# An attention order with early loads, an eviction and a maximum exchanged, and three splits of x moved one tile earlier

## What is computed

```python
scores = scale * np.matmul(q, k.transpose(0, 1, 3, 2))
scores = np.where(causal, -1000000000.0, scores)
scores = scores - scores.max(-1, keepdims=True)
a = np.exp(scores)
a /= a.sum(-1, keepdims=True) + 1e-09
local = np.matmul(a, v)
...
mem_ret = np.einsum('bhsd,bhde->bhse', q_p, M_prev)
mem_norm = np.einsum('bhsd,bhd->bhs', q_p, z_prev)[..., None] + 1e-06
mem_out = mem_ret / mem_norm
g = 1.0 / (1.0 + np.exp(-beta))[None, :, None, None]
return (g * mem_out + (1 - g) * local).astype(np.float32)
...
h = x @ w_in
g = np.where(pos, h, np.where(neg, 0.0, (h + beta) ** 2 / (4.0 * beta)))
return (g @ w_out).astype(np.float32)
...
h = x @ w_in
g = h * (1.0 / (1.0 + np.exp(-h)))
return (g @ w_out).astype(np.float32)
```

## Time and profile before

| what | value |
|---|---|
| median of the runs | 1012.22 us |
| lowest and highest | 1009.32 and 1012.91 us |
| the profiled execution | 1008.85 us |
| its span | 1006.8 us |
| granted clock of PE, mean | 0.998 |
| PE busy | 987.4 us (98%) |
| DVE, ACT, POOL busy | 486.4, 382.4, 293.7 us |

### The profile page before, as it was taken

One profiled execution on the slowest core, in us unless ns is written; L12 is line 12 of the kernel. 1 busy time (PEld: TensorE's weight loads), 2 busy tenths in 40 slices (PEclk: granted clock), 3 DMA queues, 4 the chain that ended last, 5 costly groups with the idle time before them and its releaser, 6 DMA issues.

```text
span 1006.8 us, 14060 instructions
## 1 busy us (share of the span) xinstructions
PE 987.4 (98%) x5466; PEld 819.7 (81%) x5466; DVE 486.4 (48%) x943; ACT 382.4 (38%) x831; POOL 293.7 (29%) x321
## 2 busy tenths in 40 slices
PE   7999999999999999999999988999999999999998
PEld 5777877778888888888888987888888888888897
DVE  6999889866434434443444564322332232232232
ACT  5888888733223322322222333322232232222232
POOL 6999999689300000000000699000000000000000
PEclk9999999999999999999999999999999999999999
DMA  6445455223200000000000243000000100100010
GB/s 197 140 140 149 144 154 143 70 85 115 63 0 1 1 1 1 1 1 1 0 1 1 65 130 110 1 1 22 21 1 0 42 1 1 42 1 1 1 43 21
DMA packets 38401, 48.10 MB, mean 48 GB/s; under 512 B 3264, under 2 KB 21696, under 8 KB 38336
## 3 DMA queue, kind: packets, MB, share of 16 engines
q1 hardware_dynamic: 38336, 47.20, 15.7%
HBM read 42.47 MB, written 4.72 MB: 47 GB/s over the span
## 4 chain that ended last, share of the span: by engine, by line
PE 91%; POOL 3%; DVE 3%; ACT 2%; issue 1%; DMA 0%; POOLq 0%; DVEq 0%
PE ps L946 25%; PE ps L948 25%; PE ps L947 25%; PE ps L879 4%; PE ps L824 4%; PE ps L799 3%; PE ps L898 1%; POOL W L308 1%; PE ps L811 1%; PE ps L872 1%; DVE glo L738 1%; PE ps L849 1%; PE ps L865 1%; PE ps L911 1%; PE ps L858 1%
## 5 line engine op out<-in xcount | busy, mean ns | idle before, releaser
L946 PE MATMUL ps<-xhi,W 128*128 128x512 f32 (+1 forms) x640 | 235.5, 368 | 2.7 <-POOL W L308 2.7
L947 PE MATMUL ps<-xlo,W 128*128 128x512 f32 (+1 forms) x640 | 235.4, 368 | 0.0
L948 PE MATMUL ps<-xhi,W 128*128 128x512 f32 (+1 forms) x640 | 235.4, 368 | 0.0
L738 DVE TENSOR_TENSOR glo<-act_t,ghi 128x512 fp32r<-128x512 f32 (+1 forms) x160 | 119.1, 744 | 224.8 <-ACT ghi L543 224.8
L543 ACT CAST ghi<-act_t 128x512 fp32r<-128x512 f32 (+1 forms) x160 | 92.5, 578 | 236.3 <-PE ps L948 214.4
L946 PEld LDWEIGHTS ps<-xhi,W 128*128 128x128 f32 x640 | 120.6, 188 | 23.4 <-POOL W L308 2.9
L947 PEld LDWEIGHTS ps<-xlo,W 128*128 128x128 f32 x640 | 120.6, 188 | 20.5
L306 POOL CAST W<-stage 128x512 fp32r<-128x512 f32 x64 | 47.9, 749 | 305.4 <-PE ps L948 301.1
L948 PEld LDWEIGHTS ps<-xhi,W 128*128 128x128 f32 x640 | 120.6, 188 | 20.1
L535 ACT ACTIVATE act_t<-act_t,half_col 128x512 f32<-128x512 f32 (+1 forms) x80 | 54.4, 681 | 190.8 <-DVE act_t L731 190.8
L946 PE MATMUL ps<-ghi,W 128*128 128x512 f32 (+1 forms) x320 | 118.3, 370 | 2.6 <-DVE glo L738 2.5
(11 more groups left out here) (105 smaller groups left out, 1356.4 us busy)
## 6 DMA issues: line engine op xcount, KB each, us to landing
stage<-in_moe_w_in SPq DMA_DIRECT2D x32, 256.0 KB, 2.7
stage<-in_moe_w_out SPq DMA_DIRECT2D x32, 256.0 KB, 2.6
qraw<-in_qT SPq DMA_DIRECT2D x16, 320.0 KB, 3.3
vn<-in_vN SPq DMA_DIRECT2D x16, 320.0 KB, 5.0
kraw<-in_kT SPq DMA_DIRECT2D x16, 288.0 KB, 2.8
qn<-in_qN SPq DMA_DIRECT2D x16, 288.0 KB, 5.0
zb<-in_zN SPq DMA_DIRECT2D x32, 144.0 KB, 3.5
out_x<-ostage SPq DMA_DIRECT2D x17, 256.0 KB, 2.0
```

The lines of the kernel that those rows point to most:

```text
L738: nc.vector.tensor_tensor(glo[:, f % SLOTS, 0:TN[tile]], a, ghi[:, f % SLOTS, 0:TN[tile]].bitcast(F32), ALU.subtract).then_inc(glo_done, 1)
L946: nc.tensor.matmul(dst, w_lo_, x_hi_, start=first, stop=False)
L947: nc.tensor.matmul(dst, w_hi_, x_lo_, start=False, stop=False)
L948: return nc.tensor.matmul(dst, w_hi_, x_hi_, start=False, stop=last)
```

## The change

Four things change.

- The start: the second pair's k and q are loaded into the still unused `probT`, right behind the first pair's, without a wait. The k and q semaphores are now one for each parity. The five matmuls over zeros have 256 columns, and the zeros are 256 columns wide. On DVE `low_k(1)` stands before the first maximum, `low_q(1)` after the fourth, and the gates after the ninth. On ACT the two parts of phi stand after the second and the fourth exponential; before, they stood ahead of the first and after the second. ACT waits for both low parts before it evicts into `probT`.
- From the second pair on DVE runs `rows` 0 and 1 (`den`, `rw`) before `to_x` and `empty_second`; before, after them.
- Maximum 5 stands between the evictions of T_M21 and T_M31; before, it stood after both.
- The second layer's first x is split in tile 3 at f = 14 (two parts) and 15 and in tile 4 at f = 4; before, in tile 4 alone.

```diff
-    SPLIT_AT = [(4, 5, 6, 7), (2, 6, 10, 13)]
+    SPLIT_AT = (4, 5, 6, 7)
+    FIRST_AT = ((TILES - 2, 14), (TILES - 2, 14), (TILES - 2, 15), (TILES - 1, 4))
...
+        def k_raw(p):
+            return probT[:, 0, 0, :] if p == 1 else kraw[:]
+
+        def q_raw(p):
+            return probT[:, 1].rearrange("p j s -> p (j s)")[:, 0:MAIN + P] if p == 1 else qraw[:]
...
             def load_k(p):
-                if p:
+                if p >= 2:
                     sp.wait_ge(lo_done, 2 * p - 1)
-                sp.dma_start(kraw[:], kT[p]).then_inc(k_in, 16)
+                sp.dma_start(k_raw(p), kT[p]).then_inc(k_in[p % 2], 16)
...
             load_k(0)
             load_q(0)
+            load_k(1)
+            load_q(1)
             for e in range(2):
                 sp.dma_start(braw[e * D:(e + 1) * D], bN[e:e + 1, :].broadcast_to([D, 12])).then_inc(b_in, 16)
             load_n(0)
-            load_k(1)
-            load_q(1)
...
-            phi_part_1(0)
             for c in range(2):
                 exps(0, c)
+            phi_part_1(0)
+            for c in range(2, 4):
+                exps(0, c)
             phi_part_2(0)
-            for c in range(2, NB):
+            for c in range(4, NB):
                 exps(0, c)
+            act.wait_ge(lo_done, 4)
...
-                        if f in SPLIT_AT[last] and not (last and layer):
-                            k_ = SPLIT_AT[last].index(f)
-                            if last and k_ == 0:
-                                act.wait_ge(acc_dve, ACCS * 2)
-                            split_x(layer + last, (tile + 1) % TILES, k_)
+                        if f in SPLIT_AT and not last:
+                            split_x(layer, tile + 1, SPLIT_AT.index(f))
+                        for k_, at in enumerate(FIRST_AT):
+                            if layer == 0 and at == (tile, f):
+                                if k_ == 0:
+                                    act.wait_ge(acc_dve, ACCS * 2)
+                                split_x(1, 0, k_)
...
-            nc.vector.memset(turned[:, 0, 0:BANK], 0.0).then_inc(zeros, 1)
+            nc.vector.memset(turned[:, 0, 0:2 * P], 0.0).then_inc(zeros, 1)
...
                 if p:
+                    rows(p, 0)
+                    rows(p, 1)
                     to_x(p - 1)
-                empty_second(p)
-                if p == 0:
-                    for step in range(2):
-                        norms(0, step)
-                rows(p, 0)
-                rows(p, 1)
+                    empty_second(p)
+                else:
+                    empty_second(0)
+                    norms(0, 0)
+                    norms(0, 1)
+                    rows(0, 0)
+                    rows(0, 1)
...
                 empty_main(p, T_M21, 2, 1)
+                if more:
+                    maximum(p + 1, 5)
                 empty_main(p, T_M31, 3, 1)
                 if more:
-                    for c in range(5, 8):
+                    for c in range(6, 8):
                         maximum(p + 1, c)
...
             for _i in range(WARM):
-                nc.tensor.matmul(ps[:, 7, :], turned[:, 0, 0:P], turned[:, 0, 0:BANK], start=True, stop=True)
+                nc.tensor.matmul(ps[:, 7, 0:2 * P], turned[:, 0, 0:P], turned[:, 0, 0:2 * P], start=True, stop=True)
```

48 lines of the change are left out of this document (26 added, 22 removed).

## The result

| | before | after |
|---|---|---|
| median, lowest, highest | 1012.24 (1009.32 to 1012.91) us | 999.15 (998.56 to 1000.3) us |
| ratio, with its 95% interval | | 0.9878 [0.9856, 0.9899] |
| the profiled execution, its span | 1008.85, 1006.8 us | 1000.3, 998.2 us |
| start of the first layer in that span | 208.77 | 205.72 |
| first 256-column product of the last tile to the second layer's first product | 55.46 | 49.94 |

The changed kernel is 1.2% faster: 13.1 us between the medians, but 8.55 us between the two profiled executions. The forecast was a gain of 10.35 us, to 1001.9 us. The tiles in between did not change (342.86 us from the first layer's start to the last tile before, 342.89 after), and neither did the second layer (399.75 us before, 399.65 after).

A forecast was written before the change was run, and what follows sets the result against it. PE, busy 98% of the span, bounds the kernel, so only its work, clock or 19.4 us of standing count. 6.0 + 1.9 + 2.6 - 0.15 = 10.35 us off 1012.22 gives 1001.9 us, range 997.5 to 1006.5.

The forecast's parts named there:

- last tile: End of the first layer: three of four `xlo` splits moved to tile 3 let the second layer start 6.0 us earlier.
- start: First pairs: earlier scores bring POOL's chain forward, a gain of 1.9 us, bounds 0.3 and 2.8.
- steady pairs: Before the first value matmuls: maximum 5 fills DVE's idle time, removing PE's short waits; 2.6 us, bounds 0.7 and 3.6.
- what is next late: Last tile, splits moved: DVE's chain, with `glo` held up by POOL, leaves PE 0.8 us late at f = 13.
- the last line of the sum: Whole kernel: the 10.35 us gain, worked out on the profiled execution, is taken off the median 1012.22, giving 1001.9 us.
- the gain is POOL's advance: First pairs: PE gains only what POOL's chain gains, 1.9 us, with POOL starting its sums at 10.7 likely.
- In pairs like pair 8 it fits by 0.27: Steady pairs: maximum 5 fits DVE's gap only by 0.27; eviction about 0.2 later, 0.18 us gained in six pairs.
- (a): Rival, whole kernel: only the last tile pays, POOL's chain starts late and steady gains cancel; 1005.9 us, chance 0.13.
- (b): Rival, steady pairs: `den` ahead of the eviction of x is caught by two POOL instructions; 1019.9 us, chance 0.04.
- (c): Rival, start: shorter warm-up brings the 1.2 GHz level into the first scores, cutting POOL's advance to 0.8; 1003.0 us, chance 0.10.
- no 0.5 in the clock: Start: a sign that the forecast holds, the granted clock showing no 0.5.
- (d): Rival, last tile: PE did wait for POOL's weights, so the freed `xlo` gives nothing beyond `glo`; 1004.6 us, chance 0.04.

The follow-up runs named there:

- e1: The kernel before with only the second layer's first x splits moved (three to tile 3, one at f = 4 of tile 4): 1005.17 us, ratio 0.9932.
- e8: The changed kernel, with POOL pausing after two blocks of second-layer weights until the last tile's f = 12 activations are done with: 998.21 us, ratio 0.9878.
- e3_steady: The kernel before with only the row sums ahead of `to_x` and maximum 5 between the evictions: 1009.95 us, ratio 0.9982.
- e9: The changed kernel, with POOL leaving out the weighting of the second pair's v: 999.27 us, ratio 0.9888.
- e11: The changed kernel, with POOL making the sums of phi for pairs 2 and 3 behind `widen`: 999.21 us, ratio 0.9888.
- e5: The changed kernel with row sums 0 and 1 back behind the evictions of x and T_M1: 999.51 us, ratio 0.9887.
- e2: The kernel before with only the new start (early loads, 256-column warm-up, new order of the first pair): 1007.5 us, ratio 0.9961.
- a2_after: The changed kernel run once more, unaltered, as a reference: 999.54 us, ratio 0.9889.
- e6_warm512: The changed kernel with the warm-up of 5 x 512 columns put back: 1001.08 us, ratio 0.9895.
- e4_nomax: The changed kernel with maximum 5 back behind both evictions: 1001.53 us, ratio 0.9906.
- e13_warm1: The changed kernel with one 256-column product of warm-up in place of five: 999.84 us, ratio 0.9893.

## Why the prediction came out as it did

The forecast was 1001.9 us and the range 997.5 to 1006.5; the result, 999.15, lies inside, 2.75 us under the forecast.

| term | predicted | profile to profile | alone, by the ratio |
|---|---|---|---|
| last tile | 6.0 | 5.5 | 6.9 [5.7, 8.2] |
| start | 1.9 | 1.44 | 3.9 [2.6, 5.2] |
| steady pairs | 2.6 | 1.8 | 1.8 [0.9, 2.7] |
| last pair | -0.15 | -0.16 | |

**Last tile: right, in mechanism and size.** The releaser named by the view was wrong and the timeline right: e1 removes the wait without touching POOL's weights. What the step took for what is next late, `glo` held up by POOL at 0.8 us, was 1.27 or 0.3 us by the meeting of the two; e8 shows the cause by removing it. Tile 3 took no longer. The trace gives 5.5 and 5.6 us; the 6.9 of the ratio holds scatter, or the clock that may fall behind the wait (e3_steady).

**Start: the mechanism half right, the size too small by 2 us; this is where most of the 2.75 us come from.** The step that was off is the last line of the sum: "The median of the runs is 1012.22, 3.4 above it; the prediction is of a median: 1012.22 - 10.35". It carried a gain worked out on one execution over to the median, as if the 3.4 us had nothing to do with the change. Part of them was the change's own place: in e1 and e3 the old start takes 2 us more than in the earlier trace rows, since the warm-up holds the first scores to 8.4 us. Worked out from 8.41, the scores' advance is 2.3 and not 1.3 us. The rest is luck of the first four runs: the kernel before had a median of 1012.24 in them and of 1011.13 to 1011.44 in the three later groups, against which the gain of the changed kernel is 11.6 to 12.3 us. So about 1 us of the 2.75 belongs to no part of the change as far as is shown, though the runs with the lower clock, above, may be part of it. The step on POOL was sound where the scores ran at the full pace (10.71, predicted 10.7), and the wait for `rwide` in pair 2 stayed, as foretold. But that the gain is POOL's advance was only half of it: without 1.8 us of POOL's work nothing was gained (e9), because POOL's casts then held DVE's `rw` and `rwt`, and DVE's eviction was as late as POOL's `rwide` had been. Where neither was late, PE did come 0.76 us earlier, and lost it again to the work put off (e11).

**Steady pairs: the mechanism right, one term too large.** Predicted were six pairs with the whole 0.25 us and six with 0.18. The first are there, 12.05 - 11.80. Of the other six, four gain 0.09, 12.05 - 11.96, one 0.18, and one lost 0.25 (12.30). "In pairs like pair 8 it fits by 0.27" was right, but what follows was read from one instruction ahead, not from what holds DVE up before it: `rwt` beside POOL's cast. The hope for `den` ahead of x came to nothing (e5).

**Rivals.** (a), only the last tile pays, is out by e2 and e3. (b), `den` caught twice and a slower kernel, did not occur; `den`, 1.31 us in the earlier trace rows, takes 0.80 us at the most in the 16 pairs of after. The mechanism behind (b), DVE held up by POOL, does decide things, but at `rw`, `rwt` and `glo`: `glo` takes 0.43, 0.87 or 1.55 us, and 0.43 once POOL pauses (e8). By the Trainium skill, "SBUF — State Buffer", section "Who interferes with whom", a VectorE instruction with two SBUF inputs contends with a GpSimd instruction that reads SBUF; `glo`, which reads `act_t` and `ghi`, agrees. (c), the clock, happened in five of nine profiles and cost 0 to 0.7 us by the start of pair 2's values. The sign "no 0.5 in the clock" held in just those five; the four others have a 0.50 between 13 and 22 us. (d) is out.

## What to carry to other kernels

When the profiled execution lies well below the median, find out where it was lucky before a gain is carried over: a second profile of a kernel with the same start would have shown the 2 us. Where two engines are both nearly full (POOL 12.00 and DVE 11.54 of 12.16 us in pair 2 of a2_after), look for the second chain before the first is relieved; here relief of POOL by 1.8 us was worth nothing, since its casts then met DVE's row sums, and put-off work came back as the same wait two pairs later. The smallest operations of DVE count too when they stand ahead of an eviction: beside POOL the four-column `rwt` took 0.62 us for 0.16, the nine-column `den` 1.31 for about 0.25, the 512-column `xlo` 1.78 for 0.69.

## What the runs showed of the hardware

**The pace at the start is a matter of chance.** The same instructions at the same times run at either level. In the warm-up of 512-column products the pace doubled at about 4.6 us in one profile, at 5.9 in another (e6_warm512) and at about 6.5 in two; with 256-column products it doubled at 4.3 to 6.7 us in four of nine profiles and only at 10.3 to 10.5 us in five. The Trainium skill says so too, "TensorE: Matmul & The Clock Gate", section "What's actually happening": the same kernel shows a different number of slow matmuls from run to run.

**The granted clock of a stretch does not show it.** After's stretch from 2 to 12 us reads 1.00, with products of 128 columns 0.105 us apart. The clock record in the trace has its first entry only where the pace doubles, at 10.51 us in after and at 4.31 in e8_pausepool, and the view counts what lies ahead of it as 1.00. The fall later on does show (0.50 from 14 to 16 us in e4_nomax). At the start of a span, the distance between products is the thing to read.

**A half pace early went with no dip later.** Five executions with the half pace to 10 us kept 1.00 to 24 us; the four with the full pace by 6.7 us fell to 0.50 between 13 and 22, and so did the three with the old start. e6_warm512 had neither, and e13_warm1 both, so it is no rule, and what decides it stays open.
